# Attention and mixture of experts on one core: the experts' first layer by one level of Strassen's scheme, token pairs in the outer loop

## What is computed

```python
scores = scale * np.matmul(q, k.transpose(0, 1, 3, 2)) + bias   # bias: a small MLP of the distance
attn = np.exp(scores - scores.max(-1, keepdims=True)); attn /= attn.sum(-1, keepdims=True) + 1e-09
x = np.matmul(attn, v)            # as (N, D) = (2304, 512)
logits = x @ w_gate               # (N, 8)
P = np.exp(logits - logits.max())
for _ in range(8):
    P /= P.sum(1, keepdims=True) + 1e-09
    P /= P.sum(0, keepdims=True) + 1e-09
    P *= N / E
for e in range(E):                # E = 8, w1[e] (512, 1024), w2[e] (1024, 512)
    h = np.maximum(x @ w1[e], 0.0)
    out += P[:, e:e + 1] * (h @ w2[e])
```

## Time and profile before

| | |
|---|---|
| three runs | 1995.48, 1996.52, 1997.40 us, median 1996.52 |
| profiled execution, first to last instruction | 1994.2 us (span) |
| mean granted TensorE clock | 0.997 of full speed |
| PE / DVE / ACT / POOL busy | 98 / 31 / 26 / 13% of the span |
| DMA | 84.23 MB, 42 GB/s over the span |

### The profile page before, as it was taken

One profiled execution on the slowest core, in us unless ns is written; L12 is line 12 of the kernel. 1 busy time (PEld: TensorE's weight loads), 2 busy tenths in 40 slices (PEclk: granted clock), 3 DMA queues, 4 the chain that ended last, 5 costly groups with the idle time before them and its releaser, 6 DMA issues.

```text
span 1994.2 us, 30651 instructions
## 1 busy us (share of the span) xinstructions
PE 1961.2 (98%) x10920; PEld 1714.8 (86%) x10920; DVE 611.7 (31%) x1312; ACT 523.8 (26%) x991; POOL 258.8 (13%) x120
## 2 busy tenths in 40 slices
PE   8999999799999999999999999999999999999998
PEld 4677777589999999999999999999999999999997
DVE  9777777442121212121212121212121212121211
ACT  8777777311121112111211121112111211121110
POOL 1233333200030003000300030003000300030000
PEclk9999999999999999999999999999999999999999
DMA  7754441200020002000200020002000200010000
GB/s 235 216 125 114 113 119 41 85 0 0 0 85 0 0 0 84 0 0 0 83 1 0 0 82 3 0 0 81 3 0 0 81 4 0 0 42 16 32 16 32
DMA packets 39391, 84.23 MB, mean 42 GB/s; under 512 B 9018, under 2 KB 17466, under 8 KB 37316
## 3 DMA queue, kind: packets, MB, share of 16 engines
q1 hardware_dynamic: 39364, 83.90, 14.3%
HBM read 68.55 MB, written 15.34 MB: 42 GB/s over the span
## 4 chain that ended last, share of the span: by engine, by line
PE 96%; DMA 1%; issue 1%; DVE 1%; SPq 0%; ACT 0%; POOL 0%; DVEq 0%; ACTq 0%; POOLq 0%
PE banks L535 14%; PE banks L536 13%; PE banks L537 13%; PE banks L547 13%; PE banks L548 13%; PE banks L549 13%; PE banks L445 4%; PE banks L406 3%; PE banks L388 2%; PE banks L354 2%; PE banks L389 2%; PE banks L469 1%; DMA raw<-in_qk 1%; PE banks L416 0%; DVE w_lo L827 0%
## 5 line engine op out<-in xcount | busy, mean ns | idle before, releaser
L861 DVE SCALAR_TENSOR_TENSOR h_lo<-banks,h_hi 128x384 fp32r<-128x384 f32 x384 | 214.2, 558 | 1010.2 <-ACT h_hi L669 1009.9
L535 PE MATMUL banks<-x_hi,w_hi 128*128 x1536 | 522.0, 340 | 0.3 <-DVE w_lo L827 0.3
L669 ACT ACTIVATE h_hi<-banks 128x384 fp32r<-128x384 f32 x384 | 188.7, 492 | 1269.5 <-PE banks L537 1269.5
L537 PE MATMUL banks<-x_hi,w_lo 128*128 x1536 | 517.6, 337 | 0.0
L536 PE MATMUL banks<-x_lo,w_hi 128*128 x1536 | 516.8, 336 | 0.0
L547 PE MATMUL banks<-w_hi,h_hi 128*128 128x512 f32 x1152 | 452.0, 392 | 11.8 <-DVE h_lo L861 11.8
L548 PE MATMUL banks<-w_lo,h_hi 128*128 128x512 f32 x1152 | 450.9, 391 | 0.0
L549 PE MATMUL banks<-w_hi,h_lo 128*128 128x512 f32 x1152 | 448.7, 389 | 0.0
L535 PEld LDWEIGHTS banks<-x_hi,w_hi 128*128 128x128 f32 x1536 | 288.3, 188 | 11.6 <-issue 0.4
L536 PEld LDWEIGHTS banks<-x_lo,w_hi 128*128 128x128 f32 x1536 | 288.3, 188 | 11.2
L932 POOL TENSOR_TENSOR w_lo<-stage,w_hi 128x1024 fp32r<-128x1024 f32 x57 | 136.3, 2404 | 1243.1 <-ACT w_hi L653 1236.2
(11 more groups left out here) (74 smaller groups left out, 1051.8 us busy)
## 6 DMA issues: line engine op xcount, KB each, us to landing
stage<-in_expert_w SPq DMA_DIRECT2D x64, 512.0 KB, 3.2
raw<-in_qk SPq DMA_DIRECT2D x32, 576.0 KB, 7.1
bias_scratch<-bias_out SPq DMA_DIRECT2D x36, 288.0 KB, 2.1
bias<-bias_scratch SPq DMA_DIRECT2D x16, 288.0 KB, 2.8
out<-total SPq DMA_DIRECT2D x6, 768.0 KB, 3.5
v_main<-in_v SPq DMA_DIRECT2D x16, 256.0 KB, 2.7
bias<-bias_scratch SPq DMA_DIRECT2D x16, 256.0 KB, 3.4
bias<-bias_scratch SPq DMA_DIRECT2D x4, 144.0 KB, 2.6
```

Source lines behind the costliest of these rows:

```text
L535: pe.matmul(dst, hi, xh, start=(c == 0), stop=False)
L537: mm = pe.matmul(dst, lo, xh, start=False, stop=(c == DC - 1))
L669: act.activation(h_hi[:, f % RING, :], banks[:, f % RING, 0:T], ACT.Relu).then_inc(h_rounded, 1)
L861: dve.scalar_tensor_tensor(h_lo[:, f % RING, :], banks[:, f % RING, 0:T], 0.0, h_hi[:, f % RING, :].bitcast(F32), ALU.max, ALU.subtract).t ...
```

## The change

**Order.** The outer loop now runs over three pairs of token tiles: tile p of tokens 0 to 1151 and tile p of tokens 1152 to 2303, 384 each. Inside are the eight experts, and inside each four pairs of hidden blocks (`FPAIRS`). One such unit, 768 tokens by 256 hidden units, is a *period* g; there are 96. Loops are written out (no `Fori`). Weights are therefore loaded three times, 1 MB per period, into two `stage` slots.

**Strassen.** In a period the first layer is a 2 x 2 block product (features in two halves, hidden units in two, tokens in two), and 7 products (`PRODUCTS`) take the place of 8, each 2 chunks x 3 = 6 matmuls of 384 columns into bank 0 or 1. Two pairs of products accumulate in PSUM. What is added for it:

- POOL: four sums of weight blocks per period (`sum_weights`, 256 elements each, line L1053 and on), four sums of token blocks per tile pair (`sum_factor`, 768 elements each);
- ACT and DVE: the seven token factors rounded and split per tile pair; the weights rounded and split in three parts of 768, 1024 and 1024 elements per period (`round_weights` on ACT, `split_weights` on POOL, L1064);
- ACT: a copy of product 1 (`keep_first`); DVE: five sums of bank and copy per period (`combine`), three of them into `corner`; three of the four hidden blocks are then rounded and split from `corner` in SBUF, one from PSUM.

Between two products (from the third on, with one group after the second) stands a second-layer group of the period before (`second_layer`, 6 matmuls of 512 columns, six token blocks, banks 2 to 7).

**Logits.** 72 plain fp32 matmuls after period 0's products: x (128 features x 128 tokens) as weights, the gate (8 columns) moving. The x rounding (L641) and `low_part` in attention are gone; `x` is kept in fp32.

**Normalisation.** DVE's nine half-round steps and POOL's eight reductions are spread over periods 1 to 3, three places each. The output of a tile pair is stored when it is done, the last in six pieces of 256 KB.

```diff
-    def split_weights(n, f):
-        pool.wait_ge(w_rounded, n + 1)
-        pool.tensor_tensor(w_lo[:, f], stage[:, f % RING], w_hi[:, f].bitcast(F32),
-                           ALU.subtract).then_inc(w_split, 1)
...
-    pool.partition_all_reduce(top[:, 1:2], top[:, 0:1], P, RMAX).then_inc(top_all, 1)
-    split_weights(FC - 1, FC - 1)
-    for k in range(ITERS):
-        pool.wait_ge(col_ready, k + 1)
-        pool.partition_all_reduce(col_sum[:], col_part[:], P, RADD).then_inc(col_all, 1)
+    for g in range(ALL):
+        p, at = g // PERIODS, g % PERIODS
+        for i in range(NW):
+            if g + 1 < ALL:
+                split_weights(g + 1, i)
+            if 1 <= g < 4 and 3 * (g - 1) + i < ITERS:
+                column_totals(3 * (g - 1) + i)
+        if g == 0:
+            pool.wait_ge(top_ready, 1)
+            pool.partition_all_reduce(top[:, 1:2], top[:, 0:1], P, RMAX).then_inc(top_all, 1)
+        if g + 2 < ALL:
+            sum_weights(g + 2)
+        if 4 <= at < 4 + SUMS and p + 1 < TILE_PAIRS:
+            sum_factor(p + 1, at - 4)
```

```diff
+PRODUCTS = ((0, 0, True), (4, 1, True), (1, 0, False), (5, 1, False), (3, 0, True), (2, 1, True), (6, 0, False))
...
+    def product(g, k):
+        w, which, fresh = PRODUCTS[k]
+        p = g // PERIODS
+        if g % PERIODS == 0:
+            pe.wait_ge(x_split, NP * p + k + 1)
+        if k == 0:
+            pe.wait_ge(w_split, NW * g + 2)
+            if g > 0:
+                pe.wait_ge(combined, 5 * g - 1)
+        elif k == 1:
+            if g > 0:
+                pe.wait_ge(combined, 5 * g)
+        elif k == 2:
+            pe.wait_ge(p1_kept, g + 1)
+        elif k == 3:
+            pe.wait_ge(combined, 5 * g + 1)
+        elif k == 4:
+            pe.wait_ge(h_split, 4 * g + 1)
+        elif k == 5:
+            pe.wait_ge(combined, 5 * g + 2)
+        else:
+            pe.wait_ge(combined, 5 * g + 3)
...
+    for g in range(ALL + 1):
+        for k in range(NP):
+            if g < ALL:
+                product(g, k)
+            if g > 0 and k > 0:
+                second_layer(g - 1, k - 1)
+        if g == 0:
+            logits()
```

```diff
+    for g in range(ALL):                       # DVE
...
+        combine(u2[:], product_bank(g, 1), p1_copy[:], ALU.add)
+        add_tile(g - 1, 0)
...
+        split_hidden(g, 0)
+        if 1 <= g < 4:
+            if g == 1:
+                negate_largest()
+            sinkhorn_step(3 * (g - 1))
...
+        combine(corner[:, 1, :], product_bank(g, 1), u3[:], ALU.subtract)
+        split_hidden(g, 1)
+        add_tile(g - 1, 4)
...
+        combine(corner[:, 2, :], product_bank(g, 0), u2[:], ALU.add)
+        split_hidden(g, 2)
+        if 1 <= g < 4:
+            sinkhorn_step(3 * (g - 1) + 2)
```

More of the change, by code:

```diff
@@ L64 @@
 TAIL = 6
-RING = 4
 TOK = N // P
@@ L558, in _ @@
-            with pe.Fori(0, E) as e:
-                with pe.Fori(0, TILES) as t:
-                    expert_tile(e, t)
+            def product(g, k):
[20 more added lines that the diff above has]
+                    pe.wait_ge(combined, 5 * g + 3)
+                hi, lo = w1[g % 2]
+                dst = product_bank(g, which)
+                for c in range(2):
+                    f = slice(c * P, c * P + P)
+                    pe.matmul(dst, hi[:, w, f], x_hi[:, k, c, :], start=fresh and c == 0, stop=False,
+                              skip_group_check=not fresh)
+                    pe.matmul(dst, hi[:, w, f], x_lo[:, k, c, :], start=False, stop=False,
+                              skip_group_check=not fresh)
+                    mm = pe.matmul(dst, lo[:, w, f], x_hi[:, k, c, :], start=False, stop=c == 1,
+                                   skip_group_check=not fresh)
+                mm.then_inc(product_done, 1)
@@ new lines, in logits @@
+            def logits():
+                pe.wait_ge(gate_in, 16)
+                pe.wait_ge(scaled, PIECES * X_PIECES)
+                for t in range(TOK):
+                    for c in range(DC):
+                        mm = pe.matmul(banks[:, LOGIT_BANK, E * t:E * t + E], x[:, c, t * P:t * P + P], gate[:, c, :],
+                                       start=c == 0, stop=c == DC - 1)
+                mm.then_inc(logit_done, 1)
+            for g in range(ALL + 1):
[6 more added lines that the diff above has]
+                    logits()
@@ L637, in step @@
                     round_pair(n, slot, s % QC - 1)
-                if s % QC == 0 and exists(hp, s - 10):
-                    n, slot = batch(hp, s - 10)
-                    act.wait_ge(scaled, PIECES * (n + 1))
-                    act.activation(x_piece(x_hi, n), heads[:, slot, :], ACT.Copy).then_inc(x_hi_done, 1)
             for s in range(STEPS):
@@ new lines, in _ @@
+            for k in range(NP):
+                round_factor(0, k)
+            for g in range(ALL):
+                p, at = g // PERIODS, g % PERIODS
+                more = g + 1 < ALL
+                after = at == PERIODS - 1 and more
+                keep_first(g)
+                if more:
+                    round_weights(g + 1, 0)
+                if at == 0 and p > 0:
+                    for k in range(4, NP):
+                        round_factor(p, k)
+                round_hidden(g, 0)
+                if more:
+                    round_weights(g + 1, 1)
+                if g == 1:
+                    act.wait_ge(top_neg, 1)
+                    act.activation(routing[:].rearrange("p e c -> p c e"),
+                                   banks[:, LOGIT_BANK, 0:TOK * E].rearrange("p (c e) -> p c e", e=E), ACT.Exp,
+                                   bias=top[:, 1:2]).then_inc(exp_ready, 1)
+                if after:
+                    round_factor(p + 1, 0)
+                    round_factor(p + 1, 1)
+                round_hidden(g, 1)
+                if more:
+                    round_weights(g + 1, 2)
+                if after:
+                    round_factor(p + 1, 2)
+                round_hidden(g, 2)
+                if after:
+                    round_factor(p + 1, 3)
+                round_hidden(g, 3)
@@ L891, in _ @@
+            for j in range(TJ):
+                add_tile(ALL - 1, j)
         @block.gpsimd
```

535 lines of the change are left out of this document (306 added, 229 removed).

## The result

| | before | after | forecast |
|---|---|---|---|
| median of 5 runs, us | 1997.4 (1995.5 to 1998.2) | 2005.2 (2002.0 to 2007.5) | 1985.5 |
| span of the profiled run | 1994.2 | 2005.7 (its time 2007.5) | 1983.1 |
| ratio, 95% interval | | 1.0038 (1.0025 to 1.005) | 0.994 |

What follows compares the result with a forecast made beforehand. PE bounds the kernel, busy 98%. Period 5 starts at 549.5; 91 periods of 15.58 (1417.4) and the last second layer 8.2 give 1975.1; extras make 1979.3, tail span 1983.1, median 1985.5 us; range 1966 to 2045.

Steps and rivals of the forecast that it cites:

- Part 1, fewer matmuls: Expert stage: 576 matmuls less gain 101.1 us; one period takes 15.58 us of PE.
- Part 2, does the rest fit: Expert periods: ACT 5.4, DVE 6.1, POOL 9.6 us (1.8 more in 12 periods) all fit beside 15.58 us of PE.
- Part 3, the logits: After period 0's products: 144 records at 0.11 us each take 15.8 us.
- the upper end of 22: Logits: highest of the bounds, 10 to 22 us, from records priced at about 0.07 and 0.155 us each.
- Period 0's end: Start of the expert stage: first product at 366.8, period 0's products done at 377.3 us.
- Part 4, the seam: Normalisation: POOL works in one chain with 17 switches of 6.70 or 6.93 us; sum 155.3, period 5 starts at 549.5.
- The signs that the forecast named for itself as a whole: Expert stage and its start: prediction fails as a whole if the period isn't 15.6 us or the chain isn't 155.
- The rival of the slow side, POOL keeps DVE out: Every period: DVE's corner splits wait for POOL, 1.15 x 95 = 109 us, 2095; chance 0.22, wholly or in part.
- the 1.7 from which it would show: Steady periods: DVE delay of 1.7 us, the tightest hand-over's slack, from which PE would stall.
- The small stall in every period: Expert stage: waits on more matmul groups and straight code cost 0.1 to 0.45 us each period, 1994 to 2028; chance 0.19.
- The restart: Around the seam: 4.2 us on top, 1.7 for TensorE's clock, 1.5 for period 5's hand-over, 1.0 in attention.
- The step from span to median: Whole kernel: 2.3 us added to span 1983.1 for the runs' median, carried over from the kernel before, giving 1985.5.

Runs made afterwards that it cites:

- experiment 7: Kernel before, with first- and second-layer matmul groups alternating as 6, 3, 6, 6 in five steps of a tile, same matmuls and waits; 2001.0 us (one run).
- experiment 5: Changed kernel, POOL's weight sums and splits of periods 32 to 35 cut to one column, so POOL is nearly idle at the first pair change; 2002.1 us (one run).
- experiment 4: Changed kernel, each logit matmul moving the gate eight times over, 64 columns instead of 8, same 144 weight loads; 1994.7 us (one run).
- experiments 1 and 2: First: changed kernel, eight column reductions in one row on POOL, 1942.4 us. Second: kernel before, one-column POOL addition between every two column reductions, 2065.1 us.

## Why the prediction was wrong, point by point

- **Part 1, fewer matmuls: right in kind.** 576 fewer; the period is 15.64 for 15.58. The term for the period was mis-sized by 0.4%: it took the old kernel's starts for matmuls in another form, and the second layer's 512-column matmuls start 0.2315 apart and not 0.2278. Why is open (experiment 7).
- **Part 2, does the rest fit: right for steady periods, and it was never asked for a change of the pair.** This is the first step that failed: a term of 8.1 us was put at nothing. I had DVE's splits of seven factors in the seam and none in periods 32 and 64, where three of them come again ahead of the first hidden block. At 0.95 each, near the forecast's own 0.9, they are hidden, as experiment 5 shows; with one of them held for 3.12 us beside a POOL instruction they are not. (POOL's sums of token blocks fall in 8 periods, not 12; that changes nothing in the sum.)
- **Part 3, the logits: the term that failed most.** 15.8 forecast, 27.45 measured, above the upper end of 22. The pace of a record at full clock was right (0.11, and 0.112 in experiment 4). What failed is the premise that a busy PE keeps its clock, which the sum took without saying it. I took the loss of clock only behind waits, as in the earlier trace rows. The bounds for the records came from short groups, of 3 and 4 records, in which the clock cannot be seen to fall. With 15.8 the run would have been at 1993.6 (2005.2 less 11.6, an estimate), 0.2% faster than before.
- **Period 0's end, 377.5 for 377.3: partly luck.** Attention ended 1.0 us later than before for a reason that the forecast didn't have (last section). In experiment 5's run that delay is absent, and period 0 ends at 375.4.
- **Part 4, the seam: right, 154.3 for 155.4.** POOL's switch is a price per alternation, in both directions; experiments 1 and 2 show it from both sides. The signs that the forecast named for itself as a whole, a period of 15.6 and a chain of 155, both came true; they covered neither of the terms that failed.
- **The rival of the slow side, POOL keeps DVE out: right in kind, not in place.** In steady periods the hand-over has the slack that was worked out:

```profile
1204.74 2.05 DVE L955 SCALAR_TENSOR_TENSOR h_lo<-corner,h_hi 128x384 fp32r<-128x384 f32 x1
...
1203.97 2.40 POOL L1064 TENSOR_TENSOR w_lo<-stage,w_hi 128x1024 fp32r<-128x1024 f32 x1 [3.09 <-ACT w_hi L717]
1206.33 1.06 POOL L1053 TENSOR_TENSOR stage<-stage 128x256 f32<-128x256 f32 x1
```

  DVE's split ends at 1206.79, 0.4 us behind POOL's, 1.5 us late and under the 1.7 from which it would show; after it the two take turns, POOL's sum at 1.06 for 0.73. The mean of such splits is 1158 ns in after where a split from PSUM takes 557, and behind the seam PE waits for none of them; at the changes it waits for the split from PSUM that stands behind the factors'. The Trainium skill (SBUF — State Buffer, "Who interferes with whom") has the exclusion; the rows agree with it, and they add that POOL's queue did not hold on to its turn here. The forecast gave this rival as one price for all 95 periods. What came was 8.1 us in two of them.
- **The small stall in every period: it came, at 0.06 us and not at 0.1 or more**, without a wait.
- **The verdict.** The forecast's margin of 11 us was less than the two terms that were missing or mis-sized by 8 and 12 us; with the 5.9 us of the periods they turned its sign. The restart went the other way, 2.3 us for 4.2. (The clock of 0.81 over 10 us in the earlier trace rows is 3.8 us at half speed and 1.9 us lost; the forecast's words have the 1.9 as the time at half speed, its sum as the loss.) The step from span to median was off as well: 2.3 us were added, but the profiled run of after was the slowest of five, and the median is 0.5 below its span. So the median misses by 19.7 us where the span misses by 22.6.

## What to carry to other kernels

Count how often GpSimd alternates between elementwise work and a cross-partition reduction on a chain, and multiply by 6 to 7 us (5.8 to 7.8 in these runs), whatever the size of the work: here the order alone was worth 63 us. Where PE runs many loads with few moving columns, look at the granted clock and not only at PE's busy share; more columns for nothing can be faster. Cost the rare periods (a change of tile, a restart) apart from the steady one: what hides in 90 of 96 needn't in the others.

## What the runs showed of the hardware that was not expected

- The clock fell to 0.50 with PE busy 100% of the time, in loads of 128 columns with 8 moving; with 64 moving it stayed at 1.00.
- A plain fp32 matmul of 384 columns is two records of 0.335 us each at full clock, some 4 cycles a column in all.
- DVE back to back starved POOL: at the start of after, one POOL instruction lasted from 13.83 to 62.36 us, 48.53 us, where its like takes 2.64. DVE's row beside it is 96 instructions without a gap; POOL's instruction ends 2.5 us after DVE's first pause, at 59.89:

```profile
11.46 47.09 DVE L818 TENSOR_SCALAR hidden<-table,slopes,neg_b 128x576 f32 x96
...
13.83 48.53 POOL L1037 TENSOR_TENSOR qk_hi<-raw,qk_hi 64x1152 fp32r<-64x1152 f32 x1 [12.79 <-ACT qk_hi L652]
...
65.14 2.64 POOL L1037 TENSOR_TENSOR qk_hi<-raw,qk_hi 64x1152 fp32r<-64x1152 f32 x1
```

  PE waited 4.6 us for it and attention ended 1.0 us later than before; in the kernel before the same instruction took 5.58. It isn't fixed by the order of the program: five more traces of kernels with this start show 48.2 to 48.4 us, and experiment 5's, with the same instructions up to there, 5.64; attention ends 2.1 us earlier in it than in after. In the expert stage POOL back to back let DVE in after each instruction. Why the one side starves and the other doesn't, and why not in every run, no run here tells.
